# First output layer, last 64 features: two matmul products per weight tile, with the halves added and split afterwards

## What is computed

```
x = attention(r, k, v, w, a, b)                    # 3072 x 320
h = x @ w_in                                       # 320 -> 1024
solu = h * softmax(h)
ln = (solu - mean) / sqrt(var + 1e-6) * g_ln
z = ln @ w_out                                     # 1024 -> 320, the first output layer
h2 = z @ w2_in                                     # 320 -> 2048
g = max(h2, 0) + alpha * min(h2, 0)
y = g @ w2_out                                     # 2048 -> 320
```

## Time and profile before

| | us |
|---|---|
| median of 3 runs | 1035.58 (1026.11 to 1038.79) |
| the profiled execution | 1020.41 |
| its span | 1018.6 |
| TensorE busy in the span | 931.0 (91%) |
| VectorE busy | 652.5 (64%) |
| ScalarE busy | 437.1 (43%) |
| mean granted clock of TensorE | 0.968 of full speed |

### The profile page before, as it was taken

The page is one execution under the profiler, slowest core; times in us unless marked ns, Lnnn a source line. Parts: engine busy times, 40 slices in busy tenths (PEclk is TensorE's granted clock), DMA queues, the critical chain, the costliest instruction groups (busy, mean ns, idle before and its releaser), DMA issues.

```text
span 1018.6 us, 32985 instructions
## 1 busy us (share of the span) xinstructions
PE 931.0 (91%) x14112; PEld 880.4 (86%) x14112; DVE 652.5 (64%) x1119; ACT 437.1 (43%) x892; POOL 240.4 (24%) x453
## 2 busy tenths in 40 slices
PE   3379999998999988668999999999999999999997
PEld 3368998897898988568999999999999999999987
DVE  8866788786787545666565647464655656464734
ACT  4234455444453433355343535263434434353522
POOL 8666556575654440000000000000000000000000
PEclk9697999999999999969999999999999999999999
DMA  5735666566765442341010000000000000000000
GB/s 158 130 73 144 150 139 127 119 161 169 171 140 120 100 104 86 109 141 26 2 26 24 4 27 1 27 0 26 0 26 0 26 0 26 26 0 14 1 14 14
DMA packets 144004, 67.44 MB, mean 66 GB/s; under 512 B 120028, under 2 KB 129372, under 8 KB 143884
## 3 DMA queue, kind: packets, MB, share of 16 engines
q1 hardware_dynamic: 141772, 65.53, 26.5%
q10 hardware_dynamic: 2112, 0.13, 0.2%
HBM read 45.98 MB, written 19.66 MB: 64 GB/s over the span
## 4 chain that ended last, share of the span: by engine, by line
PE 80%; DVE 8%; issue 3%; DMA 3%; POOL 2%; ACT 2%; SPq 1%; DVEq 0%; ACTq 0%; POOLq 0%
PE acc L1047 6%; PE px L342 6%; PE acc L1049 5%; PE acc L1048 5%; PE bank L1047 5%; PE bank L1049 5%; PE bank L1048 5%; PE mid L1047 4%; PE mid L1049 4%; PE mid L1048 4%; PE pq L404 4%; PE pr L355 3%; PE py L430 2%; PE mid L1100 2%; PE mid L1101 2%
## 5 line engine op out<-in xcount | busy, mean ns | idle before, releaser
L1276 POOL TENSOR_TENSOR stats<-stats 128x1 f32<-128x1 f32 x24 | 13.2, 550 | 574.9 <-DVE stats L1359 574.9
L1381 DVE SCALAR_TENSOR_TENSOR stage<-mid,w_raw 128x512 f32<-128x512 f32 x96 | 66.4, 692 | 110.0 <-ACT w_raw L1222 109.9
L1047 PE MATMUL acc<-wo_h,act_h 128*128 128x320 f32 x384 | 122.1, 318 | 6.6 <-DVE act_l L1290 6.4
L1218 ACT ACTIVATE stage<-mid 128x512 f32<-128x512 f32 x96 | 57.3, 597 | 162.2 <-PE mid L1101 162.2
L1049 PE MATMUL acc<-wo_l,act_h 128*128 128x320 f32 x384 | 119.2, 310 | 0.0
L1048 PE MATMUL acc<-wo_h,act_l 128*128 128x320 f32 x384 | 119.1, 310 | 0.0
L1047 PE MATMUL mid<-zT_h,w_h 128*128 128x256 f32 x384 | 108.8, 283 | 0.7 <-DVE zT_s L1290 0.7
L1049 PE MATMUL mid<-zT_l,w_h 128*128 128x256 f32 x384 | 108.7, 283 | 0.0
L1048 PE MATMUL mid<-zT_h,w_l 128*128 128x256 f32 x384 | 108.7, 283 | 0.0
L789 POOL TENSOR_TENSOR al<-al,prod 40x512 f32<-40x512 f32 x48 | 68.5, 1426 | 101.2 <-DMA al<-a_features_first 88.8
L1222 ACT ACTIVATE w_raw<-stage,minus_alpha 128x256 f32<-128x256 f32 x192 | 87.4, 502 | 3.1
(11 more groups left out here) (153 smaller groups left out, 2376.8 us busy)
## 6 DMA issues: line engine op xcount, KB each, us to landing
wkb<-wkb_features_first SPq DMA_DIRECT2D x46, 242.5 KB
rvu<-rv_features_first SPq DMA_DIRECT2D x48, 160.0 KB
l_scr<-lb SPq DMA_DIRECT2D x24, 256.0 KB, 4.4
x_scr<-x SPq DMA_DIRECT2D x24, 256.0 KB, 3.3
al<-a_features_first SPq DMA_DIRECT2D x48, 80.0 KB
sv<-v_time_first SPq DMA_DIRECT2D x48, 80.0 KB, 4.8
out<-y_sb SPq DMA_DIRECT2D x12, 320.0 KB, 2.3
d_scr<-s_x SPq DMA_DIRECT2D x12, 256.0 KB, 2.4
```

Source lines behind the costliest of these rows:

```text
L1047: pe.matmul(o, left[0], right[0], start=start, stop=False)
L1218: act.activation(neg[q % 2][:], mid[q % 2][:], ACT.Relu, scale=-1.0).then_inc(neg_ready, 1)
L1381: dve.scalar_tensor_tensor(out=act_f[q % 2][:], in0=mid[q % 2][:], scalar=0.0, in1=slope[q % 2][:], op0=ALU.max, op1=ALU.add).then_inc(act ...
```

## The change

The third weight tile is no longer held twice. `wo1[0]` keeps the high parts of all 320 columns and, in its last 64 columns, the low parts of the last 64 features; so one weight tile holds high and low parts side by side. `wo1[1]` now uses 256 columns. In `layer1_out` the last 64 features come first: for each `f` two matmuls with that tile, one with the high and one with the low part of the input. Partitions 0 to 63 of the result are the products with the high weights, partitions 64 to 127 those with the low weights; their sum is the value. ScalarE copies the upper half down, VectorE adds the two, ScalarE writes the high parts and VectorE the low parts, each behind a semaphore of its own. The low-by-low product is now included for these features. `z_hi_dup` goes away and a float32 tile `z_last` takes its place. Three semaphores are new. `first_high` writes 320 columns in place of 384, and `first_low` becomes two instructions, of 256 and of 64 columns, for each `f`.

```diff
-    z_hi_dup = sb("z_hi_dup", [P, 2 * P], F32R)
+    z_last = sb("z_last", [P, 2 * P])
...
-    first = [(wts["w_out"][:, f:f + 2], wo1[0][:, f:f + 2], wo1[1][:, f:f + 2]) for f in range(0, FT1, 2)]
+    first = [(wts["w_out"][:, f:f + 2], wo1[0][:, f:f + 2, 0:DM], wo1[1][:, f:f + 2, 0:2 * P],
+              wo1[0][:, f:f + 2, DM:DP]) for f in range(0, FT1, 2)]
...
             pe.wait_ge(nT_high, 4 * c + 4)
             pe.wait_ge(nT_low, 2 * c + 2)
-            for d in range(3):
+            o = banks[1][:, 512:768]
+            for f in range(FT1):
+                for part in range(2):
+                    ins = pe.matmul(o, wo1[0][:, f, 2 * P:DP], nT[part][:, f], start=f == 0 and part == 0,
+                                    stop=f == FT1 - 1 and part == 1)
+            ins.then_inc(z_done, 1)
+            for d in range(2):
...
-            high(act, first[i][1], first_raw(i)).then_inc(early_high, 1)
+            high(act, first[i][1], first_raw(i)[:, :, 0:DM]).then_inc(early_high, 1)
...
         def take_z(c):
 
+            act.wait_ge(z_done, 3 * c + 1)
+            act.copy(z_last[0:HALF], banks[1][HALF:P, 512:768]).then_inc(z_part_ready, 1)
+            act.wait_ge(z_last_ready, c + 1)
+            high(act, zTs[0:HALF], z_last[0:HALF]).then_inc(z_last_high, 1)
             act.wait_ge(z_done, 3 * c + 3)
-            high(act, zT[0][:], banks[1][:, 0:512].rearrange("p (k t) -> p k t", k=2))
-            high(act, zTs[0:64], banks[1][0:64, 512:768])
-            high(act, z_hi_dup[HALF:P], banks[1][HALF:P, 512:768]).then_inc(z_high, 1)
+            high(act, zT[0][:], banks[1][:, 0:512].rearrange("p (k t) -> p k t", k=2)).then_inc(z_high, 1)
...
-            low(dve, first[i][2], first_raw(i), first[i][1]).then_inc(early_low, 1)
+            low(dve, first[i][2], first_raw(i)[:, :, 0:2 * P], first[i][1][:, :, 0:2 * P])
+            low(dve, first[i][3], first_raw(i)[:, :, 2 * P:DM], first[i][1][:, :, 2 * P:DM]).then_inc(early_low, 1)
...
         def low_z(c):
 
+            dve.wait_ge(z_part_ready, c + 1)
+            dve.tensor_tensor(z_last[0:HALF], banks[1][0:HALF, 512:768], z_last[0:HALF], ALU.add).then_inc(z_last_ready, 1)
+            dve.wait_ge(z_last_high, c + 1)
+            low(dve, zTs[HALF:P], z_last[0:HALF], zTs[0:HALF])
             dve.wait_ge(z_high, c + 1)
-            low(dve, zT[1][:], banks[1][:, 0:512].rearrange("p (k t) -> p k t", k=2), zT[0][:])
-            low(dve, zTs[HALF:P], banks[1][HALF:P, 512:768], z_hi_dup[HALF:P]).then_inc(z_low, 1)
+            low(dve, zT[1][:], banks[1][:, 0:512].rearrange("p (k t) -> p k t", k=2), zT[0][:]).then_inc(z_low, 1)
```

More of the change, by code:

```diff
@@ L926, in feed_forward @@
     z_done, z_high, z_low = sem("z_done"), sem("z_high"), sem("z_low")
+    z_part_ready, z_last_ready, z_last_high = sem("z_part_ready"), sem("z_last_ready"), sem("z_last_high")
     mid_done, act_ready, act_high, act_low = sem("mid_done"), sem("act_ready"), sem("act_high"), sem("act_low")
```

## The result

The changed kernel takes 1017.92 us (median of 4 runs, 1014.14 to 1020.35), the kernel before 1032.89 us (median of 4, 1026.11 to 1038.79). These medians lie 15.0 us apart. The ratio of the two kernels, which the comparisons use, is 0.9879 with a 95% interval of 0.9839 to 0.9919. That is 12.5 us faster (8.4 to 16.6), within 2%. The forecast was a gain of 12.9 us and 1022.7 us.

A forecast was written before the change was run, and what follows sets the result against it. TensorE was taken to bound the kernel from chunk 1 on, so a matmul less is time less. Fewer matmuls 10.9, last chunk 0.91 and start-up 1.04 sum to 12.9 us: 1035.6 to 1022.7 us, range 1010 to 1031.

The forecast's parts named there:

- rival (a): Start-up: TensorE's clock holds after the shorter idle time, 1.1 us more gain, 14.0 in all, 1021.6 us; chance 0.30.
- Part 1: TensorE in `layer1_out`: eight matmuls less in each chunk, 0.909 us a chunk, 10.9 us in all.
- Part 2: New chain for the last 64 features and its three waits: at most 2.5 us, covered by TensorE's matmuls, cost 0.
- Part 3: Shorter end of the z path: nothing in chunks 1 to 10; last chunk's `layer2` 1.82 us earlier, 0.91 new.
- Part 4: Start-up chain to the first `acc`: 1.95 us earlier, 1.04 us of it new; TensorE's idle time 3.04 to about 2.0.
- the first link: Start-up: VectorE's low part of weight piece 11 starts 1.95 us earlier than 458.50, with all later links the same.
- Part 5: Weight preparation beside the attention: shorter ScalarE passes, two VectorE instructions a piece; taken as 0, between -0.6 and +0.6 us.
- (b): Only the removed matmuls pay, start-up and last chunk give nothing: 10.9 us gain, 1024.7 us; chance 0.13.
- The sign that failed: Whole profiled span: the forecast counts as wrong if it is not 11 to 15 us shorter.
- (c): New matmuls in `layer1_out`: reusing a weight tile costs time, at worst 25 us slower, 1061 us; chance 0.02.
- (d): Hand-overs outlast their 5.4 us cover, or TensorE waits for `act_l` elsewhere: about nothing left, 1033 to 1036 us; chance 0.05.

The follow-up runs named there:

- two_last: Changed kernel with the last 64 features computed last, so their chain stands at the end of the z path; ratio 0.9907 to the kernel before, 9.6 us faster.
- chain_longer: Changed kernel with five unused VectorE reductions of 1024 columns in the new chain of every chunk, between add and low part; executed once, 1025.37 us.
- order_only: Kernel before with the last 64 features first in `layer1_out`, no matmul removed, weights still held twice; ratio 0.995 to the kernel before, 5.1 us faster.
- apart: Changed kernel with the 16 new matmuls reordered so no weight tile is used twice in a row; executed once, 1020.81 us; 46.31 us a chunk.
- idle_longer: Changed kernel with one unused VectorE reduction of 1024 columns in the start-up, after the split of the last weight piece; executed once, 1016.20 us.
- after_again: Changed kernel without any edit, for a second profile; ratio 0.9861 to the kernel before, 14.3 us faster.
- before_again: Kernel before without any edit, for a second profile; 572.2 us from the start of `layer1_out` to the end, against 573.3 in the first profile.
- piece11_early: Changed kernel with weight piece 11 split earlier in the start-up, in the pause before `zT_h` of chunk 0; ratio 0.9833 to the kernel before, 17.2 us faster.

## Why the prediction was right

**The sum.** By the means of the two profiles of each kernel, the part from the start of `layer1_out` on is 13.7 us shorter: 1.1 up to `zT_h` of chunk 0, 1.2 from there to the first `acc`, 1.3 from there to `zT_h` of chunk 1, 9.0 over the ten chunk distances, and 1.0 in the rest. The forecast was 12.9, and 14.0 with rival (a).

**Part 1** was right and carries the gain: 0.903 us a chunk measured, 0.909 forecast; 9.03 us over chunks 2 to 11. What was left out, the lower clock in chunk 0, is real: the distance to `zT_h(0)` is 9.95 to 11.11 us with 72 matmuls and 8.94 to 10.31 with 64 (two_last aside, where the chain stands in it). Multiplied by the mean granted clock of that stretch (0.74 to 0.84, and 0.71 to 0.83), it is 8.2 to 8.4 us and 7.3 to 7.4. So the eight matmuls are worth 0.9 us there too, and the wandering is the moment at which the clock rises. The Trainium skill's formula ("TensorE: Matmul & The Clock Gate", section "Back-to-back issue gap"), which that section calls the gap of an isolated matmul and the prediction called that of a stream, gives 109 ns; the 114 ns measured for the new matmuls are above it as well.

**Part 2** was right: no cost. Forecast at most 2.5 us for the chain and over 2 us of slack; measured from 921.46 to 923.71, 2.3 us with the wait for VectorE, and 3.2 us of slack. In the two profiles of the changed kernel `zT_s` is finished at least 2.1 us before `zT_h` starts, in every chunk. chain_longer shows that 5.7 us more would still cost nothing in the middle chunks.

**Part 3** was right. From the start of the last `layer1_out` to the first `mid` behind it were 980.89 - 970.04 = 10.85 us, and are now 974.72 - 965.69 = 9.03: 1.82 us, as forecast.

**Part 4** was right in kind and a little too small: 14.1 to 14.3 us became 12.9 to 13.1, 1.24 us by the means for 1.04 forecast. Comparing before with after, the first link gave nearly what was forecast: VectorE began piece 11 1.36 us behind `zT_h` (463.81), for 2.45 before, 1.09 us less. Another 0.12 came where it was not looked for: the maximum followed the last piece that much closer.

**Part 5**: in the changed kernel VectorE takes 0.69 and 0.29 us for a piece, for 0.95 before. Their durations overlap: the next piece starts 0.81 us behind the first. Whether that moves the attention could not be seen beside its own wandering.

**The clock.** Between the forecast and rival (a) the forecast took the wrong side: the idle time of 1.64 to 1.82 us did not let the clock fall, and the case that came is (a). Its size was overrated: 1.1 us were put in for a fall of the clock, 0.3 to 0.5 are measured. VectorE's timeline shows why a lost clock costs so little there; before, and after:

```profile
474.39 0.69 DVE L1290 TENSOR_TENSOR act_l<-stage,act_h 128x512 fp32r<-128x512 f32 x1
```

```profile
479.56 0.69 DVE L1300 TENSOR_TENSOR act_l<-stage,act_h 128x512 fp32r<-128x512 f32 x1
```

This is the `act_l` of the second pair. It starts 4.05 us behind the first `acc` in both (470.34 and 475.51), whatever the clock. At full clock TensorE is there early, waits 0.98 us and begins the second pair 4.88 us behind the first; at the lower clock it begins it after 5.26 us without a wait.

**The base.** Forecast from the median of three runs, 1035.6. The median of 24 runs of the kernel before in the experiments was 1030.0. The measured 1017.9 is 4.8 us below the forecast; 2.7 of these are the base (1035.6 to 1032.9), the rest is rival (a) and the spread of the runs. The range of 1010 to 1031 would have held for (a) and (b) as well: what tells them apart is the trace, not the time.

**The sign that failed.** The spans of the first pair of profiles differ by 6.3 us, not 11 to 15. The prediction's own reading that the gain lies in TensorE's stream held; what it left out is that the attention changes by up to 10.5 us from one execution to the next. The distance from the start of `layer1_out` to the end would have been the right sign.

Rivals (b), (c) and (d) have fallen: by order_only (b), by apart and the 0.114 us between the new matmuls (c), by the table's chunk distances (d).

## What to carry to other kernels

On an engine that never waits, an instruction less is worth its distance to the next start, not its listed duration, and it is worth that everywhere; a shorter path behind it is worth something only where the next stage has no other work before it, here in the start-up and the last chunk. Look at these two places separately, and look there for an engine that stands still while it holds up a load. When part of the kernel wanders from execution to execution, cut the profiles at a common event and compare the pieces, and put the signs of being wrong on such a piece too.

## What was not expected of the hardware

The attention of one and the same kernel took 10.5 us more in one execution than in another (445.28 and 455.74), with granted clocks of 1.00 and 0.87 from 350 to 400 us. That window holds only a part of it: the 21st of the 24 `lower` of VectorE starts at 363.52 and at 370.92, so 7.4 us were lost by then. Nor does the window decide on the length: in idle_longer the clock is 1.00 there and the start is at 453.63. Ten profiles, whose attention differs at most in the preparation of a few weights, spread from 445 to 460. In the start-up, idle times of 1.64 to 1.82 us left the clock at 1.00 in four of four profiles (after, after_again, order_only, apart); 2.88 to 3.61 us let it fall in five of five (before, before_again, two_last, idle_longer, chain_longer). In all nine the clock had been at 1.00 ahead of the gap. What decides on the clock in the attention was not tried and stays open: from 350 to 400 us no idle time of TensorE is over 1.25 us, and the clock is 0.85 in one profile (piece11_early) and 1.00 in two (before, idle_longer).
